# Top-32 attention scores selected on the larger and the smaller of two half-rows, with the mask before the exponential

## The reference

```python
scores = scale * np.matmul(q, k.transpose(0, 1, 3, 2))        # 4 batches, 8 heads, 576 x 576
kth = np.partition(scores, -32, axis=-1)[..., -32:-31]
scores = np.where(scores >= kth, scores, -1000000000.0)
scores = scores - np.max(scores, axis=-1, keepdims=True)
attn = np.exp(scores)
attn = attn / (np.sum(attn, axis=-1, keepdims=True) + 1e-09)
x = heads_side_by_side(np.matmul(attn, v))                    # 2304 tokens x 512
h = np.maximum(np.maximum(x @ w1, x @ w2), x @ w3)            # 2304 x 768
x = h @ w_out
# then: expert = argmax of x @ w_gate + bias; out = gate * relu(x @ w1[e]) @ w2[e]
```

## Time and profile before

| what | value |
|---|---|
| median of 3 runs | 1110.03 us (1108.11 to 1115.01) |
| the profiled execution: its time, its span | 1106.57 us, 1105.0 us |
| TensorE busy in the span | 958.0 us (87%) |
| VectorE busy | 830.1 us (75%) |
| ScalarE busy | 674.0 us (61%) |
| GpSimd busy | 429.2 us (39%) |
| mean granted TensorE clock | 0.960 of full |

### The profile page before, as it was taken

How to read it: one execution, slowest core, us unless ns; L and a number is a source line. 1 busy time by engine, 2 the same in 40 slices (tenths; PEclk the granted TensorE clock), 3 DMA queues, 4 the chain that set the end, 5 groups by cost and what they waited for, 6 DMA issues and landing times. The chain is left out here.

```text
span 1105.0 us, 17854 instructions
## 1 busy us (share of the span) xinstructions
PE 958.0 (87%) x5708; PEld 751.1 (68%) x5709; DVE 830.1 (75%) x1677; ACT 674.0 (61%) x1557; POOL 429.2 (39%) x576
## 2 busy tenths in 40 slices
PE   5467879999999999999999999988964299999996
PEld 2145667767777687767777687767852199987995
DVE  5999999999999999999999999995214331133120
ACT  2688877877798787977798787975211222242221
POOL 1255534554355534554355534555051222211221
PEclk9987999999999999999999999999987599999998
DMA  3621111111112211111111111110000551111100
GB/s 118 227 63 36 51 51 50 51 47 54 48 50 52 63 42 46 56 56 51 50 47 55 60 46 46 38 32 21 10 1 19 181 190 48 38 47 38 48 29 28
DMA packets 58304, 63.09 MB, mean 57 GB/s; under 512 B 8176, under 2 KB 42096, under 8 KB 58224
## 3 DMA queue, kind: packets, MB, share of 16 engines
q1 hardware_dynamic: 54304, 52.63, 15.6%
q0 software_dynamic: 3920, 9.48, 2.7%
HBM read 53.28 MB, written 9.60 MB: 57 GB/s over the span
## 5 line engine op out<-in xcount | busy, mean ns | idle before, releaser
L772 PE MATMUL m_ps<-xT,w_sb 128*128 128x192 f32 x1728 | 305.6, 331 | 3.8 <-ACT xT L590 3.8
L680 DVE MAX8 top<-work 128x8 f32<-128x576 f32 x432 | 299.9, 758 | 0.0
L772 PEld LDWEIGHTS m_ps<-xT,w_sb 128*128 128x128 f32 x1728 | 278.1, 190 | 27.6 <-issue 22.0
L682 DVE MATCH_REPLACE8 work<-top,work 128x576 f32<-128x576 f32 x288 | 212.2, 755 | 0.0
L513 POOL TENSOR_TENSOR probs<-probs,exps 128x576 f32<-128x576 f32 x144 | 201.8, 1417 | 0.0
L504 POOL TENSOR_SCALAR probs<-probs,half_inv 128x576 f32<-128x576 f32 x144 | 118.4, 827 | 179.4 <-DVE half_inv L650 179.4
L718 PE MATMUL s_ps<-k_sb,q_sb 64*128 64x288 f32 (+1 forms) x768 | 143.6, 474 | 35.8 <-ACT scores L575 19.9
L731 PE MATMUL t_ps<-ident,probs 128*128 128x128 f32 x720 | 108.2, 282 | 36.9 <-ACT probsT L584 33.7
L731 PEld LDWEIGHTS t_ps<-ident,probs 128*128 128x128 f32 x720 | 83.6, 144 | 75.1 <-issue 59.5
L536 ACT ACTIVATE probs<-scores,top 128x576 f32<-128x576 f32 x144 | 111.8, 777 | 21.0 <-DVE top L680 21.0
L584 ACT COPY probsT<-t_ps 128x640 f32<-128x640 f32 x192 | 102.5, 560 | 33.5 <-PE t_ps L731 31.7
(11 more groups left out here) (138 smaller groups left out, 1187.9 us busy)
## 6 DMA issues: line engine op xcount, KB each, us to landing
k_sb<-keys_t SPq DMA_DIRECT2D x48, 288.0 KB, 2.9
v_sb<-values SPq DMA_DIRECT2D x48, 256.0 KB, 2.6
raw<-e_w SPq DMA_DIRECT2D x8, 1024.0 KB, 8.4
q_sb<-queries_t SPq DMA_DIRECT2D x48, 96.0 KB, 1.9
w_sb<-w SPq DMA_DIRECT2D x3, 1536.0 KB, 12.3
maxout_rows<-x_rows SPq DMA_DIRECT2D x18, 256.0 KB, 2.0
v_sb<-values SPq DMA_DIRECT2D x48, 32.0 KB, 2.6
wo_sb<-w_out SPq DMA_DIRECT2D x1, 1536.0 KB, 16.9
```

Of the source, the lines that this page charges most:

```text
L680: nc.vector.max(best, src).then_inc(topk_step, 1)
L682: nc.vector.match_replace(work[:, i, :], best, src, LOWEST).then_inc(topk_step, 1)
L772: ins = nc.tensor.matmul(dst[:, a * BLK:(a + 1) * BLK], w_sb[:, w, c, (first + a) * P:(first + a + 1) * P], xT[:, b % 2, c, :], start=(c = ...
```

## The change

**Scores.** For tiles 0 and 1, Q0 multiplies by the second half of the keys, and Q1 by the first half minus the second, which GpSimd makes (`key_differences`). Q1 thus gives the difference of the two scores of a pair. ScalarE copies Q0, and from Q1 takes the positive part (`rise`) and the negative part (`fall`). GpSimd (`fold`) makes `upper` = second + rise, the larger of each pair, `lower` = second - fall, the smaller, and restores the first half. Tile 2 is as before.

**Selection.** The best 32 of `upper` (288 wide, 7 steps) and the best 16 of `lower` (288 wide, 3 steps) replace the 7 steps on 576 for tiles 0 and 1. Two small reductions on VectorE, of minima and then of their maximum, give the 32nd best (`kth`).

**Softmax.** GpSimd turns all scores below `kth` into very negative ones in place (`leave_out`: L546 makes 0 or -1e9, L560 adds it). ScalarE then makes one exponential with its sum, and after VectorE's `full_sums` and `inverses` one division (`divide`), in round r + 1. The steps on ScalarE are 7, dealt out by `SOFTMAX_AT`. GpSimd's loop becomes: mask round r - 1, key differences of round r + 3, fold round r + 2.

**Order.** `round_items` puts H0 right behind Q1, and H1 right behind Q2, with groups between. The choosing and counting of experts come a round earlier.

```diff
@@ -47,12 +47,19 @@
...
-SOFTMAX_SPAN = 0.75
...
+TOP_STEP = 2
+SMALL_CHAIN = 3
+FOLDED = 2
+FOLD_BUFS = 3
...
 WORK = {"Q": 1.2, "H": 0.8, "V": 1.8, "A": 2.7, "X": 5.3, "T": 0.5, "L": 0.9}
-INVERSE_AT, INVERSE_LAG = 0, 2
+SOFTMAX_AT = (0.0, 0.2, 0.38, 0.56, 0.78, 0.86, 0.94)
+INVERSE_AT = 4
 TOP_BUFS = 3
-MAXOUT_AT = (1, 2)
+MAXOUT_AT = 2
+CHAIN_STEPS = CHAIN * GROUP + SMALL_CHAIN * FOLDED
@@ -122,7 +129,7 @@
...
-CHOOSE_AT, COUNT_AT = ROUNDS + 1, ROUNDS + 2
+CHOOSE_AT, COUNT_AT = ROUNDS, ROUNDS + 1
@@ -140,18 +147,20 @@
...
-    first, second = -(-len(groups) // 3), -(-2 * len(groups) // 3)
+    third = len(groups) - len(groups) // 3 if len(groups) > 2 else len(groups) - 1
+    second = max(third - -(-len(groups) // 3), 0) if len(groups) > 1 else third
...
-    items = [q[0], v] + groups[:first] + [q[1]] + groups[first:second] + [h[0], q[2], h[1]] + groups[second:] + [h[2]]
+    start = [v] + groups[:second] if (r - FIRST_PART) % RPB == 0 else groups[:second] + [v]
+    items = [q[0]] + start + [q[1], h[0]] + groups[second:third] + [q[2], h[1]] + groups[third:] + [h[2]]
...
-def softmax_share(items, steps):
...
-    return [min(steps, int(np.ceil(steps * w / (SOFTMAX_SPAN * work[-1])))) for w in work]
+    return [w / work[-1] for w in work]
@@ -376,6 +392,22 @@
...
+        def best_eight(r, i, chunk):
+            last = TOP_STEP * TOPK - TOP_STEP
+            first = last - TOP_STEP * MAX8 * chunk
+            stop = first - TOP_STEP * MAX8
+            return top[:, r % TOP_BUFS, i, first:stop if stop >= 0 else None:-TOP_STEP]
...
+        def best_eight_lower(r, i, chunk):
+            first = TOP_STEP * (MAX8 * chunk + 1) + 1
+            return top[:, r % TOP_BUFS, i, first:first + TOP_STEP * MAX8:TOP_STEP]
...
+        def kth_of(r, i):
+            return kth[:, r % TOP_BUFS, i:i + 1] if i < FOLDED else top[:, r % TOP_BUFS, i, 0:1]
@@ -450,7 +482,33 @@
...
+            def key_differences(r):
+                slot = r % 2
+                pool.wait_ge(qk_in[slot], (r // 2 + 1) * 32)
+                if r >= 2:
+                    wait_apart(pool, passed, scores_ready, (r - 2) * GROUP + 2)
+                nc.gpsimd.tensor_tensor(k_diff[:, slot, :], k_sb[:, slot, 0:HALF], k_sb[:, slot, HALF:SEQ],
+                                        ALU.subtract).then_inc(k_diff_ready, 1)
...
+            def fold(r):
+                slot, ring = r % FOLD_BUFS, r % RING
+                wait_apart(pool, passed, scores_copied, r * GROUP + 2)
+                if r >= FOLD_BUFS:
+                    wait_apart(pool, passed, topk_step, (r - FOLD_BUFS + 1) * CHAIN_STEPS)
+                second = scores[:, ring, 0:FOLDED, HALF:SEQ]
+                nc.gpsimd.tensor_tensor(upper[:, slot, :, :], second, rise[:, :, :], ALU.add).then_inc(fold_step, 1)
+                nc.gpsimd.tensor_tensor(lower[:, slot, :, :], second, fall[:, :, :], ALU.subtract).then_inc(fold_step, 1)
+                pool.wait_ge(fold_step, r * 3 + 1)
+                nc.gpsimd.tensor_tensor(scores[:, ring, 0:FOLDED, 0:HALF], upper[:, slot, :, :], fall[:, :, :],
+                                        ALU.subtract).then_inc(fold_step, 1)
+            key_differences(0)
@@ -481,40 +539,34 @@
...
-            def one_round(r):
...
+            def leave_out(r):
...
+                def below(i):
+                    nc.gpsimd.tensor_scalar(masked[:, i % 2, :], scores[:, r % RING, i, :], kth_of(r, i), MASKED,
+                                            ALU.is_lt, ALU.mult).then_inc(mask_ready, 1)
+                wait_apart(pool, passed, fold_step, (r + 1) * 3)
+                wait_apart(pool, passed, kth_ready, r + 1)
+                below(0)
                 for i in range(GROUP):
+                    if i == 1:
+                        wait_apart(pool, passed, masked_ready, r * GROUP + 1)
                     if i + 1 < GROUP:
-                        mask(i + 1)
+                        below(i + 1)
                     pool.wait_ge(mask_ready, r * GROUP + i + 1)
...
+                    nc.gpsimd.tensor_tensor(scores[:, r % RING, i, :], scores[:, r % RING, i, :], masked[:, i % 2, :],
+                                            ALU.add).then_inc(masked_ready, 1)
+            for r in range(-AHEAD, ROUNDS + 1):
+                if r >= 1:
+                    leave_out(r - 1)
+                if in_range(r + AHEAD + 1):
+                    key_differences(r + AHEAD + 1)
+                if in_range(r + AHEAD):
+                    fold(r + AHEAD)
@@ -525,54 +577,47 @@
...
-                def first_sign(i):
...
-                        act.wait_ge(topk_step, (r + 1) * (CHAIN * GROUP))
...
                 def shifts():
...
+                    act.wait_ge(kth_ready, r + 1)
+                    nc.scalar.mul(shift[:, top_slot, :], top[:, top_slot, :, TOP_STEP * TOPK - TOP_STEP], -SCALE)\
+                      .then_inc(shift_ready, 1)
...
                 def exp(i):
...
                         act.wait_ge(shift_ready, r + 1)
...
+                    wait_apart(act, passed, masked_ready, r * GROUP + i + 1)
+                    nc.scalar.activation(probs[:, r % PROB_BUFS, i, 0:SEQ], scores[:, r % RING, i, :], ACT.Exp,
                                          bias=shift[:, top_slot, i:i + 1], scale=SCALE,
...
+                                         accum_out=sums[:, slot, i:i + 1]).then_inc(exps_done, 1)
+                def divide(i):
+                    if i == 0:
+                        act.wait_ge(inverses_ready, r + 1)
+                    part = probs[:, r % PROB_BUFS, i, 0:SEQ]
+                    nc.scalar.activation(part, part, ACT.Copy, scale=inverse[:, slot, i:i + 1]).then_inc(probs_ready, 1)
+                return [shifts] + [lambda i=i, f=f: f(i) for f in (exp, divide) for i in range(GROUP)]
...
             def copy_scores(r, i):
                 act.wait_ge(scores_ready, r * GROUP + i + 1)
-                if i < 2:
-                    dst = scores[:, r % RING, 0:2, i * HALF:(i + 1) * HALF]
+                part = s_ps[:, :, 0:HALF]
+                if i == 0:
+                    nc.scalar.copy(scores[:, r % RING, 0:FOLDED, HALF:SEQ], part).then_inc(scores_copied, 1)
+                elif i == 1:
+                    if r > 0:
+                        act.wait_ge(fold_step, r * 3)
+                    nc.scalar.activation(rise[:, :, :], part, ACT.Relu)
+                    nc.scalar.activation(fall[:, :, :], part, ACT.Relu, scale=-1.0).then_inc(scores_copied, 1)
                 else:
-                    dst = scores[:, r % RING, i, :].rearrange("p (h n) -> p h n", h=2)
-                nc.scalar.copy(dst, s_ps[:, :, 0:HALF]).then_inc(scores_copied, 1)
+                    nc.scalar.copy(scores[:, r % RING, i, :].rearrange("p (h n) -> p h n", h=2), part)\
+                      .then_inc(scores_copied, 1)
@@ -617,11 +662,11 @@
...
-                for item, share in zip(items, softmax_share(items, len(steps))):
...
+                for item, done in zip(items, work_done(items)):
+                    while ran < len(steps) and SOFTMAX_AT[ran] < done:
+                        steps[ran]()
+                        ran += 1
@@ -642,12 +689,16 @@
...
+            def full_sums(r):
...
+                dve.wait_ge(exps_done, (r + 1) * GROUP)
+                nc.vector.tensor_scalar(sums[:, r % 2, :], sums[:, r % 2, :], EPS, None, ALU.add).then_inc(sum_step, 1)
+            def inverses(r):
+                dve.wait_ge(sum_step, r + 1)
+                nc.vector.reciprocal(inverse[:, r % 2, :], sums[:, r % 2, :]).then_inc(inverses_ready, 1)
...
             def one_round(r):
-                slot, units = r % TOP_BUFS, finished_units(r - 1)
...
+                    if in_range(r - 1):
+                        full_sums(r - 1)
+                        inverses(r - 1)
...
+                wait_apart(dve, passed, fold_step, r * 3 + 3)
                 wait_apart(dve, passed, scores_copied, r * GROUP + GROUP)
+                slot, steps = r % FOLD_BUFS, [r * CHAIN_STEPS]
+                def select(k, src, dst, best, before):
+                    if k > 0:
+                        wait_apart(dve, passed, topk_step, before)
+                    if k % 2 == 0:
+                        nc.vector.max(best, src).then_inc(topk_step, 1)
+                    else:
+                        nc.vector.match_replace(dst, best, src, LOWEST).then_inc(topk_step, 1)
+                    steps[0] += 1
+                    return steps[0]
+                upper_at, lower_at, full_at = [0] * FOLDED, [0] * FOLDED, 0
                 for k in range(CHAIN):
...
+                    for i in range(FOLDED):
+                        part = upper[:, slot, i, :]
+                        upper_at[i] = select(k, part, part, best_eight(r, i, k // 2), upper_at[i])
+                        if k == INVERSE_AT + 1 and i == 0 and r >= 1:
+                            inverses(r - 1)
```

(22 more changed lines are left out.)

117 lines of the change are left out of this document (33 added, 84 removed).

## The result

The change made the kernel slower: 1176.72 us median of four runs (1174.69 to 1177.98) against 1109.17 (1108.11 to 1115.01), ratio 1.060, 95% interval 1.056 to 1.064. Forecast were 1093 and a range of 1070 to 1112.

What follows compares the result with a forecast made beforehand. VectorE was taken to bound attention, with TensorE close behind and setting the pace after the change. Loss 4.3 and gains 9, 7 and 5 gave about 17 off 1106.6, 1089.6, plus 3.5 to the median: 1093 us, range 1070 to 1112.

Steps and rivals of the forecast that it cites:

- masks 3 x (0.82 + 1.4): GpSimd's two mask passes for three tiles: 6.7 us of its 11.6 us a round.
- this ring alone holds nothing up: Chain full_sums, kth, masks, exponentials: 3.6 + 6.9 + 0.9 = 11.4 us, below VectorE's round of 13.1.
- Both signs: Forecast wrong if, in eight rounds, TensorE's busy time falls clearly below 119 us or ScalarE waits over a few us.
- Start: Rounds up to 5: later begin and GpSimd waiting for round 4's keys; 104.3 us against 99.96, loss 4.3.
- Rounds 6 to 13: First rounds with maxout: TensorE and VectorE near each other, 114 us against 123.11, gain 9.
- Rounds 14 to 45: Steady rounds: each eight take 123 us against 124.5; four times 1.5 to 2, gain 7.
- Behind round 45: Rounds 46 to 49: new order covers about half of TensorE's gaps, gain 5; after them nothing.
- VectorE's round of 13.1: VectorE's work per round after the change: 13.1 us, 14.5 with a maxout, 1.4 less than before.
- rival C: Half-length VectorE passes cost their whole length without overlap: round 15.1 us, about 1134 us; chance 0.08.
- Rival A: Coupling: hand-overs cost more and V waits 4 us, eight rounds take 125; about 1104 us; chance 0.20.
- Rival B: TensorE isn't full and can give way: eight rounds take VectorE's 113.1 us; about 1052 us; chance 0.08.
- Rival D: ScalarE's 7.68 us wait behind attention may move or go as the list's writing shifts; about 1085 us; chance 0.12.

Runs made afterwards that it cites:

- a_nosum: Kernel after without VectorE's pass that adds EPS to the sums, reciprocals waiting for the exponentials themselves; ratio 1.032 to the kernel before.
- m_fast: Kernel after with each mask's first GpSimd pass as (mult, add) with zero operands, so nothing is masked; 1093.88 us, ratio 0.986.
- m_fast_nosum: m_fast (nothing is masked) also without VectorE's pass that adds EPS to the sums; ratio 0.971 to the kernel before.
- b_order: Kernel before with only the new order of the round's items (new `round_items`); 1106.07 us, ratio 0.997.
- m_both: Kernel after with the mask's penalty made on ScalarE, key differences behind the fold, and no EPS pass; 1077.55 us, ratio 0.971.
- b_slow: Kernel before with its GpSimd mask pass as (is_lt, mult) in place of (mult, add), at the old place; 1119.35 us, ratio 1.007.

## Why the prediction was wrong

**The step that failed** is the price of GpSimd's masks: "masks 3 x (0.82 + 1.4)". The 0.82 was read from a row with the same engine, shape and kind of instruction, but with (mult, add); the change's pass is (is_lt, mult), which no row of the trace showed. It takes 2.21 us. The text took no bounds for it, although it did so for the half-length selection. From it followed "masks of its three tiles are ready 3.2, 5.4 and 6.9 us after `kth`", measured 6.2, 10.0 and 11.3 in the trip above, and "11.4, below 13.1, so this ring alone holds nothing up", measured 16.9.

**The ring had two terms more** than its sum named. With 2.21 us it would have given 11.4 + 3 x 1.39 = 15.6, and 16.8 was measured. Means of the steady rounds: `kth` to the last mask 11.3 us (6.9 + 4.2 = 11.1 reckoned), then 0.7 until the last exponential starts behind the Relu copies in ScalarE's order (nothing reckoned; 1.2 in the trip above), 0.9 for the exponential, and 3.9 from the sums to `kth` for 3.6. In the last term is the held sums pass, 0.70 where 0.1 was reckoned; without it `a_nosum` took 16.1.

The held pass costs outside the ring too. In rounds 3 to 5 of `m_fast` VectorE waits for nobody, and the rounds take 14.3 us instead of 13.1 by the sums' pass alone, which takes 1.3 us there; without it they take 13.1. Busy time over two of these rounds, VectorE's is the third number after the length, 28.49 of 28.70 us, the rest are gaps of under 0.1 us each:

```profile
67.10:95.80 28.70, 16.99 (x104) 10.89 (x105) 28.49 (x85) 18.16 (x39) 22.87 (x20) 0.82 0.17 49
```

Both signs that the prediction had named for being wrong came in the kernel after, in the eight rounds from 376.5 to 501 us: TensorE busy for 115.33 us, and ScalarE waiting 34.9 us for masks (in total, times, longest):

```profile
ACT probs L593 <- POOL scores L560: 34.9, 16, 4.1
DVE sums L696 <- ACT probs L593: 13.2, 7, 3.4
```

**What was right** shows in the runs with a quick pass. Ends of VectorE's last selection in a round, and spans:

| | round 5 | round 13 | round 45 | span |
|---|---|---|---|---|
| before | 100.1 | 223.2 | 721.2 | 1105.0 |
| after | 122.7 | 256.8 | 795.0 | 1175.0 |
| `m_fast` | 109.8 | 227.6 | 720.6 | 1095.1 |
| `m_fast_nosum` | 106.8 | 220.1 | 703.5 | 1071.4 |

- Start: loss 4.3 forecast; 9.7 in `m_fast`, 6.7 without the sums pass. The stall behind the keys was there (23.5 us for round 2); missing was the 1.2 us in each of the next rounds. Why it is 6.7 even without them is open.
- Rounds 6 to 13: 114 forecast, gain 9; 117.8 in `m_fast`, 113.3 in `m_fast_nosum`.
- Rounds 14 to 45: gain 7 forecast (491 us), 5.0 in `m_fast` (493.0); 483.4 in `m_fast_nosum`, whose chip was 0.6% quicker.
- Behind round 45: gain 5 forecast, 9.3 in `m_fast`. What gave the rest is open; the order of the items isn't it, since in `b_order` this part is 383.2 us against 383.8.
- Sum of `m_fast`: -9.7 + 5.3 + 5.0 + 9.3 = 9.9 us less than before, 17 forecast. That its 1093.9 us lie so near the 1093 is in part luck: terms that cancel.
- VectorE's round of 13.1 (14.5 with a maxout): exact, by the rounds of `m_both` and `m_fast_nosum` in which VectorE never waits (13.13 and 14.52). Starts 0.36 apart, so rival C is out.
- Rival A (coupling, a round of 15.6): in kind it is what happened, by 16.8 and for another price. Rival B (TensorE isn't full): no; with quick masks and no sums pass VectorE's own eight rounds would take 113, and they take 8 x 15.13 = 121. TensorE is busy there for 121.45 of 124.50 us; that its weight loads are busy for only 92.90 gave no room. Rival D: the wait behind attention stayed, at most 8.7 us in the kernel after. The only priced way to be slower than before was C, with 0.04 left for slowdowns without a name; a slower mask was not among the rivals.

## What to carry to other kernels

A duration is good for an instruction only if the row has the same engine, shape, operation or pair of operations, and operands; where one of them differs, give it bounds, and multiply the upper one through the ring before you call the ring harmless. Compare each ring of waits with the round by a sum that has every hand-over and what stands ahead in each queue: the slow pass costs little beside the ring (`b_slow`, 0.7% for 4.4 us a round) and 83 us, over 7%, inside it (1176.7 against 1093.9). When no engine is full, take load off one that isn't in the ring and chain off the ring, one at a time: the two runs tell at once which of them holds. The version to use is `m_both`: half-length selection, the penalty by ScalarE, the fold ahead of the key differences, no EPS pass.
